# The loops of the down layer in a whole pass, turned around: token tiles outside, f tiles inside

## What is computed

```
attention   q, k, v: (4, 8, 576, 64); softmax(q k^T / 8) v within chunks of 64 tokens
            -> x: 2304 tokens x 512
MoE         P = softmax-like routing of x @ w_gate (2304 x 8), balanced by 8 Sinkhorn steps
            out = sum over 8 experts of P[:, e] * (relu(x @ w1[e]) @ w2[e]),  w1[e]: 512 x 1024
ELU layer   h = x @ w_in (512 x 2048);  g = where(h > 0, h, exp(min(h, 0)) - 1);  out = g @ w_out
```

## Time and profile before

| | us |
|---|---|
| median of three runs | 2164.53 |
| lowest, highest | 2163.47, 2165.15 |
| the profiled execution, its own time | 2163.2 |
| its span, first to last instruction | 2161.4 |
| PE busy in the span | 2130.3 (99%) |
| PEld (weight loads, beside PE) | 1937.2 (90%) |
| DVE busy | 823.4 (38%) |
| ACT busy | 455.9 (21%) |
| mean granted TensorE clock | 0.994 |

### The profile page before, as it was taken

The page is one execution under the profiler, slowest core; times in us unless marked ns, Lnnn a source line. Parts: engine busy times, 40 slices in busy tenths (PEclk is TensorE's granted clock), DMA queues, the critical chain, the costliest instruction groups (busy, mean ns, idle before and its releaser), DMA issues.

```text
span 2161.4 us, 30934 instructions
## 1 busy us (share of the span) xinstructions
PE 2130.3 (99%) x11248; PEld 1937.2 (90%) x11248; DVE 823.4 (38%) x1439; ACT 455.9 (21%) x882; POOL 22.4 (1%) x29
## 2 busy tenths in 40 slices
PE   6999999999999999999999999999999999999999
PEld 5888899999999999999999999999999989999998
DVE  3444443332333233333333332333233345555544
ACT  3333311111111111111111111111111133223222
POOL 0000003000000000000000000000000000000000
PEclk8999999999999999999999999999999999999999
DMA  5223100000000100000000001000000000000001
GB/s 126 60 59 97 40 20 20 20 20 20 19 19 19 39 19 19 19 19 19 19 19 19 19 19 35 23 19 19 19 19 19 19 20 20 20 20 20 0 30 58
DMA packets 81304, 61.39 MB, mean 28 GB/s; under 512 B 58480, under 2 KB 58480, under 8 KB 81264
## 3 DMA queue, kind: packets, MB, share of 16 engines
q1 hardware_dynamic: 79680, 58.73, 9.0%
q10 hardware_dynamic: 1584, 2.11, 0.3%
HBM read 56.12 MB, written 4.72 MB: 28 GB/s over the span
## 4 chain that ended last, share of the span: by engine, by line
PE 96%; DVE 2%; issue 1%; ACT 1%; DMA 0%; ACTq 0%; SPq 0%; DVEq 0%; POOL 0%; POOLq 0%
PE down_ps L360 29%; PE up_ps L327 22%; PE ab_ps L360 14%; PE ab_ps L327 11%; PE cd_ps L327 11%; PE down_ps L346 2%; PE cd_ps L407 2%; PE up_ps L317 2%; PE cd_ps L385 1%; PE ab_ps L399 1%; PE ab_ps L413 1%; DVE row_max L665 1%; DVE x_row L682 0%; DVE soft L668 0%; PE cd_ps L480 0%
## 5 line engine op out<-in xcount | busy, mean ns | idle before, releaser
L513 ACT ACTIVATE h_hi<-up_ps 128x384 fp32r<-128x384 f32 x204 | 100.4, 492 | 1002.9 <-PE up_ps L327 955.9
L770 DVE SCALAR_TENSOR_TENSOR acc<-down_ps,route,acc 128x512 f32 x168 | 123.9, 751 | 424.0 <-PE down_ps L360 418.4
L651 DVE SCALAR_TENSOR_TENSOR h_lo<-up_ps,h_hi 128x384 fp32r<-128x384 f32 x204 | 113.8, 558 | 301.3 <-ACT h_hi L513 301.3
L360 PE MATMUL down_ps<-w_hi_b,h_lo 128*128 128x512 f32 x480 | 187.7, 391 | 0.0
L360 PE MATMUL down_ps<-w_lo_b,h_hi 128*128 128x512 f32 x480 | 187.4, 390 | 0.0
L360 PE MATMUL down_ps<-w_hi_b,h_hi 128*128 128x512 f32 x480 | 186.9, 389 | 0.0
L360 PE MATMUL down_ps<-w_hi_a,h_lo 128*128 128x512 f32 x432 | 169.0, 391 | 0.0
L360 PE MATMUL down_ps<-w_hi_a,h_hi 128*128 128x512 f32 x432 | 169.0, 391 | 0.0
L360 PE MATMUL down_ps<-w_lo_a,h_hi 128*128 128x512 f32 x432 | 168.7, 391 | 0.0
L327 PE MATMUL up_ps<-x_hi,w_lo_b 128*128 x480 | 161.1, 336 | 0.0
L327 PE MATMUL up_ps<-x_hi,w_hi_b 128*128 x480 | 161.0, 335 | 0.0
(11 more groups left out here) (144 smaller groups left out, 4279.9 us busy)
## 6 DMA issues: line engine op xcount, KB each, us to landing
stage<-in_moe_w SPq DMA_DIRECT2D x30, 1024.0 KB, 5.0
q_raw<-in_q SPq DMA_DIRECT2D x36, 128.0 KB, 2.4
k_raw<-in_k SPq DMA_DIRECT2D x36, 128.0 KB, 2.8
v_raw<-in_v SPq DMA_DIRECT2D x36, 128.0 KB, 2.9
out<-acc SPq DMA_DIRECT2D x18, 256.0 KB, 2.0
stage<-in_moe_w_in SPq DMA_DIRECT2D x4, 1024.0 KB, 5.0
stage<-in_moe_w_out SPq DMA_DIRECT2D x4, 1024.0 KB, 5.1
stage<-in_moe_w ACTq DMA_DIRECT2D x2, 1024.0 KB, 8.8
```

The lines of the kernel that those rows point to most:

```text
L360: mm = nc.tensor.matmul(y_ps[j], h, w, start=f == 0 and n == 0, stop=f == FT - 1 and n == 2)
L513: nc.scalar.activation(h_hi[:, f, :], bank, ACT.Relu).then_inc(h_hi_done, 1)
L651: nc.vector.scalar_tensor_tensor(h_lo[:, f, :], bank, 0.0, h_hi[:, f, :].bitcast(F32), ALU.max, ALU.subtract).then_inc(h_lo_done, 1)
L770: nc.vector.scalar_tensor_tensor(acc_tile(t), y_ps[j], route_flat[:, bass.ds(EXPERTS * t + expert, 1)], acc_tile(t), ALU.mult, ALU.add).th ...
```

## The change

Where `down` is called for all four f tiles, the loop over the token tiles j is put outside and the one over f inside. The waits for h_lo_done all stand in the part of j = 0: before f = 0, 1, 2 and 3, with three matmuls between one and the next. down_done is raised after the last matmul of each j, that is after 12, 24 and 36 matmuls. A call with fewer than four f tiles (pass 16) keeps the loops as they were. Nothing else is changed.

```diff
                 if 0 in hidden:
                     pe.wait_ge(w_lo_done, PIECES * v + PIECES)
                     pe.wait_ge(acc_done, TPB * s)
-                for f in hidden:
-                    pe.wait_ge(h_lo_done, FT * s + f + 1)
-                    for j in range(TPB):
+                if len(hidden) < FT:
+                    for f in hidden:
+                        pe.wait_ge(h_lo_done, FT * s + f + 1)
+                        for j in range(TPB):
+                            for n, (h, w) in enumerate(down_terms(par, f, j)):
+                                mm = nc.tensor.matmul(y_ps[j], h, w, start=f == 0 and n == 0, stop=f == FT - 1 and n == 2)
+                            if f == FT - 1:
+                                mm.then_inc(down_done, 1)
+                    return
+                for j in range(TPB):
+                    for f in range(FT):
+                        if j == 0:
+                            pe.wait_ge(h_lo_done, FT * s + f + 1)
                         for n, (h, w) in enumerate(down_terms(par, f, j)):
                             mm = nc.tensor.matmul(y_ps[j], h, w, start=f == 0 and n == 0, stop=f == FT - 1 and n == 2)
-                        if f == FT - 1:
-                            mm.then_inc(down_done, 1)
+                    mm.then_inc(down_done, 1)
```

## The result

The changed kernel takes 2181.32 us (median of 4 runs, 2180.43 to 2182.00); the kernel before, with one more run, 2164.00 us. The ratio is 1.008, with a 95% interval of 1.0062 to 1.0097: 17.3 us slower. The profiled execution took 2181.59 us, with a span of 2179.8 us, and it is 18.4 us longer in its span than the one before.

The account below looks back on a forecast made before the run. TensorE, 96% of the chain of waits, was taken to bound the kernel. Stalls of 17.7 us less 0.1 at the end give 17.6; 2163.2 + 17.6 = 2180.8, as a median 2182 us (0.8% slower), range 2176 to 2190.

Parts of the forecast that it names:

- the end of the run: After the last matmul: the last addition no longer stands behind the one before, and the last store follows it, -0.1 us.
- The stall of f = 3: ELU blocks, f = 3: h_lo 0.82 us late, plus hand-over 0.06 and restart 0.11, loses 0.99 us per block.
- How many: 18 ELU blocks of passes 17 to 19: 17 at 0.99 us and the first at 0.91, together 17.7 us.
- MoE blocks: 90 blocks, passes 1 to 15: h_lo of f = 3 has 0.51 us margin after hand-over, so no stall.
- Rival A: MoE blocks stall too, TensorE's queue no longer far ahead: up to 0.11 us each, +9.9 us, 2192; chance 0.10.
- Banks: Fewer bank changes in `down` taken as 0 us, with bounds of -4.3 to +4.3 us over 108 blocks.
- Rival B: Bank changes cost more than starts show, 972 fewer: not slower, 2158 us at 25 ns each; chance 0.04.
- Rival C: ELU stall smaller than its parts: early h_hi terms or start surplus absorbed, 0.7 us back, 2181; chance 0.02.
- Rival D: Clock falls to 1.2 GHz in the ELU stalls, slowing nine matmuls after each: +37 us, 2219; chance 0.02.

## Why the prediction was right

The mechanism was right, one stall per ELU block from a late h_lo, and so were the number of blocks and, to 0.02 us, the price of one. Three small things were off: these 0.02 us, one block taken for another kind, and the end of the run. Their errors partly cancel.

**The stall of f = 3.** Right in place, releaser and size. The gap of 0.82 us and the hand-over of 0.06 gave 0.88, and the changed kernel shows 0.88. The restart was taken as 0.11 from a matmul of 384 columns, and a matmul of 512 shows 0.11 (0.34 less 0.23). What was left out is 0.02 us in the matmuls behind it: the nine after the stall take 2.17 to 2.19 us, 0.13 to 0.15 more than 2.04. So 1.01 per block and not 0.99.

**How many.** The count of 18 was right, but the first of the two blocks in the earlier trace rows was not one of them. The row at 1853.44 is of the sixth block of pass 16, which has no transposes in it and so looks like a whole pass in the timeline; the changed kernel runs it at L361, the branch with the old order. All 18 blocks are alike (1.015 us each to the third place), and the sum is 18 x 1.015 = 18.3 us where 17.7 was forecast. Together with the 0.02 us above this makes 0.6 us too little, and the end of the run, below, was 0.3 too much: by the measured parts the sum is 18.3 - 0.4 = 17.9 us, where 17.6 was forecast. That the two errors have opposite signs is luck. The measured 17.3 (the changed kernel) and 18.0 (the ELU passes alone) lie on either side; the start of the run alone scatters by over 1 us (last paragraph).

**MoE blocks.** Right: the margin of 0.51 us held in all 90. Rival A is out, as a mechanism too: with the margin brought down to nothing the loss is 0.02 us, and a full stall comes only with a longer chain. One sign was read wrong: the additions were to start 2.7, 5.4 and 8.2 us after the block's first matmul, which is when the last matmul of each bank is through by the distances of starts. In the block shown above (first matmul at 1014.42) they start after 3.3, 6.0 and 8.7 us. The gap between them, 2.7 us, is as forecast, and nothing hangs on the rest.

**Banks.** Right, at zero and not merely within the bounds: 16.547 us per MoE block with 12 groups and with three. Rival B is out, and none of the windows over passes 2 to 19 shows the clock below 1.00 in either order. The Trainium skill (TensorE: Matmul & The Clock Gate, section "A second HAM failure mode: psum-queue depth-cycling") tells of brief idle times between groups of matmuls that go through the banks by turns; in the MoE passes here TensorE is busy for 1390.00 of 1390 us in either order, so there is nothing for that account to work on.

**The surplus and the clock.** Rival C's small part did not come: the surplus of 0.04 us at a block's start stays and the stall comes on top. Rival D is out: at 18 waits of this length the clock stays at 1.00, and the matmuls after a wait come at 0.23 us.

**The end of the run.** This step was wrong, and small: 0.4 us where 0.1 was forecast, and by another way. I took 0.1 us off because the last addition would no longer stand behind the one before. It did not move: it starts 0.54 us after the last matmul's start before and 0.55 after. TensorE's result reaches VectorE later than I assumed:

```profile
2175.97 0.39 PE L370 MATMUL ab_ps<-w_hi_b,h_lo 128*128 128x512 f32 x1
```

```profile
2176.52 0.69 DVE L774 TENSOR_TENSOR acc<-ab_ps,acc 128x512 f32 x1 [2.03 <-PE ab_ps L370]
```

The last matmul ends at 2176.36 by the profile, the addition starts 0.16 us later; I had used the 0.06 of the way from VectorE to TensorE. Yet the tail is 0.4 us shorter: from the start of the last matmul to the end of the span it is 4.2 us before (2157.18 to 2161.4) and 3.8 after (2175.97 to 2179.8). It is 4.2 or 4.3 in each of the four experiments with the old order in the last pass and 3.8 or 3.9 in the four with early additions there. Here the rows of SyncE's queue show why. First the kernel before, then the changed one:

```profile
2157.26 2.09 SPq L269 DMA_DIRECT2D out<-acc  x3
```

```profile
2154.44 23.30 SPq L269 DMA_DIRECT2D out<-acc  x6
```

Each row reaches from the start of the first issue to the end of the last, and one issue takes 0.34 us. So the last store is issued at 2159.01 before and at 2177.40 after, and the span ends 2.4 us later in both. Before, the three additions end 0.7 us apart (2157.07, 2157.73 and 2158.41), but SyncE issues the three stores 0.87 to 0.88 us apart (2157.26, 2158.14, 2159.01), so that the last comes 0.60 us after its addition. The same distance of 0.88 us stands between the two stores of the close additions in the run with f = 3 later (2155.96, 2156.84). After, the additions are 2.7 us apart, and the last store comes 0.19 us after its addition (2177.21). The difference of 0.41 us is the whole gain: the prediction let the last store follow the last addition and left out the pace of this queue. The other runs agree. From the start of the last matmul to the issue of the last store it is 1.83 or 1.84 us in the four with the old order in the last pass, and 1.42 or 1.43 in the four with early additions there.

**The rest of the 18.4 us.** The two profiled executions differ by 0.55 us before the first changed block (its first matmul at 267.86 and at 268.41), in the attention stage and pass 0, where the code is the same in both. The experiments scatter there as well: in those without a longer MoE chain, the first matmul of `down` in pass 2 starts between 368.08 and 369.36, against 368.55 before and 369.10 after. So 0.55 + 18.3 - 0.4 = 18.4 us, up to rounding.

## What to carry over

When loops are turned around on an engine that is busy all the time, list for each operand when it is ready and at which instruction it is now needed; the loss is the gap, plus the hand-over, plus a restart, and all of it but 0.02 us per stall could be read from the trace before. An order that finishes one output first pulls the need for the last input forward (here from 6.2 to 2.1 us), and only pays if something waits for the early outputs; here nothing did but the last store, by 0.4 us. If early outputs are wanted, put the late input's matmuls behind those of a second output, as the run with f = 3 later does.

## What I had not expected

- An operand that is done 0.05 us before its weight load is due, so that the release reaches TensorE just when it is due, costs 0.02 us. TensorE needs no lead to speak of beyond the hand-over.
- Two stalls in one block cost no more than the later one. With relu(-x) twice, f = 2 stalls (0.19 us idle) and f = 3 stalls (1.22 us idle), and the loss of 1.98 us is what f = 3 alone would give.
- The first nine matmuls of a `down` take 0.04 us more than any later nine, whatever the order, the number of bank changes and the places of the waits (where a stall follows, it comes on top). What it is stays open.
